# Expert phase of a routed MLP: two tiles of one expert taken together, their up product with channels on partitions

## The reference

```python
def _moe2_ref(x, expert_emb, tau, w1, w2):
    # N, D, E, F = 3072, 384, 8, 1024
    xn = x / (norm(x) + 1e-6);  en = expert_emb / (norm(expert_emb) + 1e-6)
    logits = xn @ en.T / tau
    expert_idx = np.argmax(logits, axis=1)
    gate_w = softmax(logits)[arange(N), expert_idx]
    for e in range(E):
        mask = expert_idx == e
        h = np.maximum(x[mask] @ w1[e], 0.0)
        out[mask] = gate_w[mask, None] * (h @ w2[e])
```

## Time and profile before

| what | value |
|---|---|
| median of 3 runs | 976.58 us (976.44 to 978.68) |
| the profiled execution | 976.46 us, its span 974.7 us |
| granted clock of TensorE, mean | 0.961 |
| TensorE busy | 862.5 us (88%) |
| VectorE, ScalarE, GpSimd busy | 661.7, 464.9, 503.7 us |
| expert phase | from 657.1 us (first transposes of x) to the end |

### The profile page before, as it was taken

The page is one execution under the profiler, slowest core; times in us unless marked ns, Lnnn a source line. Parts: engine busy times, 40 slices in busy tenths (PEclk is TensorE's granted clock), DMA queues, the critical chain, the costliest instruction groups (busy, mean ns, idle before and its releaser), DMA issues.

```text
span 974.7 us, 18389 instructions
## 1 busy us (share of the span) xinstructions
PE 862.5 (88%) x6398; PEld 766.3 (79%) x6399; DVE 661.7 (68%) x1058; ACT 464.9 (48%) x859; POOL 503.7 (52%) x884
## 2 busy tenths in 40 slices
PE   1658897889989999999999999839999999999995
PEld 1435786778879888888898889828888888888785
DVE  5968897889898998999876664276232343556621
ACT  5775754645645666655454432134232333456531
POOL 1294989699998988889890000012222223233221
PEclk9968999999999999999999999968999999999998
DMA  9201152343424243231411110345311141416310
GB/s 314 91 20 30 46 142 70 87 112 90 117 70 104 86 127 83 76 86 57 109 44 46 39 38 20 140 155 202 128 42 32 48 163 41 170 43 224 104 42 31
DMA packets 41799, 89.36 MB, mean 92 GB/s; under 512 B 6248, under 2 KB 23664, under 8 KB 40416
## 3 DMA queue, kind: packets, MB, share of 16 engines
q1 hardware_dynamic: 37632, 76.04, 25.3%
q0 software_dynamic: 4096, 12.40, 4.0%
HBM read 69.55 MB, written 17.69 MB: 90 GB/s over the span
## 4 chain that ended last, share of the span: by engine, by line
PE 60%; DVE 21%; ACT 7%; issue 7%; DMA 3%; SPq 2%; DVEq 0%; POOL 0%; ACTq 0%; POOLq 0%
PE mm L1597 7%; PE mm L1601 6%; PE mm L1598 6%; PE yu L1597 5%; PE tr L1597 4%; PE tr L1601 4%; PE tr L1598 4%; PE yu L1598 4%; PE yu L1601 4%; PE mm L1837 3%; PE sc L1654 3%; PE yu L1695 2%; DVE l_im L1099 2%; DVE l_re L1098 2%; DVE h_sb L1118 2%
## 5 line engine op out<-in xcount | busy, mean ns | idle before, releaser
L1597 PE MATMUL mm<-up_hi,x_hi 128*128 128x384 f32 x432 | 157.7, 365 | 30.5 <-DVE h_sb L1118 14.8
L1598 PE MATMUL mm<-up_lo,x_hi 128*128 128x384 f32 x432 | 148.2, 343 | 0.0
L1917 POOL TENSOR_TENSOR c_re<-ring 112x128 f32<-112x128 f32 x165 | 97.5, 591 | 79.8 <-DVE ring L1071 48.0
L1995 POOL DMA_INDIRECT out_rows<-g_o,rows_out x30 | 34.7, 1155 | 179.7 <-DVE g_o L1514 179.7
L1918 POOL TENSOR_TENSOR c_im<-ring 112x128 f32<-112x128 f32 x165 | 120.4, 730 | 0.0
L1597 PEld LDWEIGHTS mm<-up_hi,x_hi 128*128 128x128 f32 x432 | 82.3, 190 | 46.3 <-DVE h_sb L1118 18.1
L958 ACT ACTIVATE g_h<-tr 128x512 f32<-128x512 f32 x60 | 35.9, 598 | 171.3 <-PE tr L1601 169.8
L1601 PE MATMUL mm<-up_hi,x_lo 128*128 128x384 f32 x432 | 100.5, 341 | 0.0
L1921 POOL TENSOR_TENSOR ring<-c_re,c_im 112x64 f32<-112x64 f32 x165 | 98.4, 596 | 0.0
L1973 POOL DMA_INDIRECT g_in<-x_scratch,rows_in x33 | 37.3, 1130 | 102.1 <-DVE rows_in L1463 77.6
L1920 POOL TENSOR_TENSOR ring<-c_re,c_im 112x64 f32<-112x64 f32 x165 | 80.3, 486 | 12.9
(11 more groups left out here) (244 smaller groups left out, 2111.0 us busy)
## 6 DMA issues: line engine op xcount, KB each, us to landing
raw<-in_moe_w SPq DMA_DIRECT2D x16, 1536.0 KB, 8.8
a_dn<-in_a_laid SPq DMA_DIRECT2D x18, 384.0 KB, 6.8
an_scratch<-a_dn SPq DMA_DIRECT2D x18, 384.0 KB, 2.3
ring<-an_scratch SPq DMA_DIRECT2D x18, 384.0 KB, 5.5
q_in<-in_q_laid SPq DMA_DIRECT2D x24, 224.0 KB, 3.1
k_in<-in_k_laid SPq DMA_DIRECT2D x24, 224.0 KB, 3.2
v_in<-in_v_laid SPq DMA_DIRECT2D x24, 192.0 KB, 3.3
x_scratch<-x_sb SPq DMA_DIRECT2D x24, 192.0 KB, 2.5
```

What stands on the lines that cost most here:

```text
L1597: nc.tensor.matmul(out, hi[:, x, :], w_hi(x), start=(x == 0), stop=False)
L1598: nc.tensor.matmul(out, hi[:, x, :], w_lo(x), start=False, stop=False)
L1917: nc.gpsimd.tensor_tensor(c_re[:, 0:count, :, :], cur, bc(prev[:, :, 0, :], 2, 2), ALU.mult).then_inc(chain_prod, 1)
```

## The change

An expert's tiles are taken in pairs; a tile left over, an expert of one tile and tile 0 are taken by `single`, which is the tile of before with another read-ahead. A pair of tiles t and t+1:

- TensorE computes h transposed: the stationary operand is a block of 128 channels of w1 and the moving one the x of both tiles, 256 columns. 8 blocks x 9 matmuls write 4 banks (`tr` and `mm`). h then has its channels on partitions, as the down product wants it, so h isn't transposed. The down product is made per tile, into `ub` and `yb`.
- ScalarE writes `gh_hi` with the Relu straight out of the bank, VectorE makes `gh_lo` with the maximum and the subtraction in one instruction. 4 of each per pair.
- Both x must be ready when a pair begins. `gx_hi` and `gx_lo` hold two tiles, `g_x` two banks, and x is read two tiles ahead. In a single, the second tile's x is copied to the first place, on ScalarE and on VectorE.
- GpSimd's step for tile t is now: gather tile t+3, wait for its landing and post `g_here`, then `store_tile(t)`.
- The gates product moves ahead of tile 0, since the one-hot tiles' memory is used again by the tiles of x and h.

The diff, cut to its core:

```diff
@@ ScalarE
-            def expert_tile(t, split=None):
+            def single(t, split=None, very_first=False):
...
-                gx_high(t + 1)
+                if very_first:
+                    gx_high(1, 1, 0)
+                    gx_high(2, 0, 1)
+                else:
+                    nc.scalar.activation(gx_hi[:, :, 0, :], gx_hi[:, :, 1, :].bitcast(F32), ACT.Copy).then_inc(high_passed, 1)
+                    act.wait_ge(high_passed, t)
+                    gx_high(t + 2, 1, 1)
...
+            def pair(t, split=None):
+                act.sem_inc(gh_ready, 4)
+                act.sem_inc(high_passed, 2)
+                for b in range(4):
+                    act.wait_ge(gh_done, 2 * t + b + 1)
+                    if b == 0:
+                        act.wait_ge(go_done, t)
+                    nc.scalar.activation(gh_hi[:, 2 * b:2 * b + 2, :, :].rearrange("p k s t -> p (k s t)"),
+                                         (tr if b < 2 else mm)[:, b % 2, :], ACT.Relu).then_inc(ghh_ready, 1)
...
+                gx_high(t + 2, 0, 0)
+                gx_high(t + 3, 1, 1)
@@ VectorE
+            def scale(t, y):
+                dve.wait_ge(go_done, t + 1)
+                dve.wait_ge(go_free, t + 1)
+                nc.vector.tensor_scalar(g_o[:, ds(t % 2, 1), :].rearrange("p t d -> p (t d)"), (ub, yb)[y][:, 0:HD], table_gate[:, ds(t, 1)], None, ALU.mult) \
+                    .then_inc(go_ready, 1)
...
+            def pair(t, split=None):
+                dve.sem_inc(low_passed, 2)
+                gx_move(t + 2, 0, t + 2)
+                if split is not None:
+                    split_lo(split, 0)
+                for b in range(4):
+                    if b == 2:
+                        gx_move(t + 3, 1, t + 2)
+                    dve.wait_ge(ghh_ready, 2 * t + b + 1)
+                    part = slice(2 * b, 2 * b + 2)
+                    nc.vector.scalar_tensor_tensor(gh_lo[:, part, :, :].rearrange("p k s t -> p (k s t)"), (tr if b < 2 else mm)[:, b % 2, :], 0.0,
+                                                   gh_hi[:, part, :, :].rearrange("p k s t -> p (k s t)").bitcast(F32), ALU.max, ALU.subtract) \
+                        .then_inc(ght_ready, 1)
+                gx_low(t + 2, 0, 0)
+                gx_low(t + 3, 1, 1)
+                if split is not None:
+                    split_lo(split, 1)
+                    split_lo(split, 2)
+                scale(t, 0)
+                if split is not None:
+                    split_lo(split, KX)
+                scale(t + 1, 1)
+                if split is not None:
+                    split_lo(split, KX + 1)
@@ TensorE
+            def pair(t, e, x_slot, new):
...
+                pe.wait_ge(ght_ready, 2 * t)
+                pe.wait_ge(gxh_ready, t + 2)
+                pe.wait_ge(gxt_ready, t + 2)
+                x_hi, x_lo = (tile[:, :, :, :].rearrange("p k s t -> p k (s t)") for tile in (gx_hi, gx_lo))
+                for f in range(KG):
+                    out = (tr if f < 4 else mm)[:, f // 2 % 2, f % 2 * 2 * P:(f % 2 + 1) * 2 * P]
+                    rows = slice(f * P, (f + 1) * P)
+                    for x in range(KX):
+                        w_hi, w_lo = (tile[:, x_slot, x, rows] for tile in (e1_hi, e1_lo))
+                        nc.tensor.matmul(out, w_hi, x_hi[:, x, :], start=(x == 0), stop=False)
+                        nc.tensor.matmul(out, w_lo, x_hi[:, x, :], start=False, stop=False)
+                        last = nc.tensor.matmul(out, w_hi, x_lo[:, x, :], start=False, stop=(x == KX - 1))
+                    if f % 2 == 1:
+                        last.then_inc(gh_done, 1)
+                pe.sem_inc(ght_done, 4)
+                fetch_x(t + 2, 0, t + 2)
+                fetch_x(t + 3, 1, t + 2)
+                pe.wait_ge(go_ready, t)
...
+                for y in range(2):
+                    product((ub, yb)[y][:, 0:HD], gh_hi[:, :, y, :], gh_lo[:, :, y, :], lambda x: e2_hi[:, slot, x, :], lambda x: e2_lo[:, slot, x, :], KG,
...
@@ GpSimd
                 held(g_fetched[x], 16 * (pair + 1))
                 pool.sem_inc(g_here, 1)
-                held(gx_moved, t + 1)
-                fetch_tile(t + 2, x)
+
+            def fetch_next(t, x):
+                held(gx_moved, t - 1)
+                fetch_tile(t, x)
...
             def expert_tile(t, pair, x):
-                pass_on(t + 1, pair + x, 1 - x)
+                fetch_next(t + 3, 1 - x)
+                pass_on(t + 3, pair + x + 1, 1 - x)
                 store_tile(t, pair, x)
```

More of the change, by code:

```diff
@@ L1526, in expert @@
-                with dve.If(end - begin > 1):
-                    with dve.Fori(begin + 1, end) as t:
-                        expert_tile(t)
-            gx_move(0)
-            gx_low(0)
+                split = e + 1 if not isinstance(e, int) else None
+                count = end - begin
+                with dve.If(count > 1):
+                    pair(begin, split)
+                    with dve.If(count > 3):
+                        with dve.Fori(begin + 2, end - 1, 2) as t:
+                            pair(t)
+                    with dve.If(count % 2 > 0):
+                        last = dve.value_load(tiles_i[0:1, 2, ds(e, 1)], min_val=1, max_val=SLOTS - 4)
+                        single(last)
@@ L1532, in _ @@
+                with dve.If(count < 2):
+                    single(begin, split)
+            gx_move(0, 0, 0)
+            gx_low(0, 0, 0)
             for n in range(KX, PIECES):
                 split_lo(0, n)
-            expert(0)
+            end = dve.value_load(tiles_i[0:1, 1, 0:1], min_val=1, max_val=SLOTS - 3)
+            single(0, 1, very_first=True)
+            with dve.If(end > 2):
+                with dve.Fori(1, end - 1, 2) as t:
+                    pair(t)
+            with dve.If((end + 1) % 2 > 0):
+                last = dve.value_load(tiles_i[0:1, 2, 0:1], min_val=1, max_val=SLOTS - 4)
+                single(last)
@@ new lines, in expert @@
+            def expert(e, x_slot):
+                begin = pe.value_load(tiles_i[0:1, 0, ds(e, 1)], min_val=1, max_val=SLOTS - 4)
+                end = pe.value_load(tiles_i[0:1, 1, ds(e, 1)], min_val=1, max_val=SLOTS - 3)
+                count = end - begin
+                with pe.If(count > 1):
+                    pair(begin, e, x_slot, True)
+                    with pe.If(count > 3):
+                        with pe.Fori(begin + 2, end - 1, 2) as t:
+                            pair(t, e, x_slot, False)
+                    with pe.If(count % 2 > 0):
+                        last = pe.value_load(tiles_i[0:1, 2, ds(e, 1)], min_val=1, max_val=SLOTS - 4)
+                        single(last, e, False)
+                with pe.If(count < 2):
+                    single(begin, e, True)
@@ new lines, in _ @@
+            pe.wait_ge(tiles_ready, 1)
+            fetch_x(0, 0, 0)
+            end = pe.value_load(tiles_i[0:1, 1, 0:1], min_val=1, max_val=SLOTS - 3)
+            single(0, 0, True, very_first=True)
+            with pe.If(end > 2):
+                with pe.Fori(1, end - 1, 2) as t:
+                    pair(t, 0, 0, False)
+            with pe.If((end + 1) % 2 > 0):
+                last = pe.value_load(tiles_i[0:1, 2, 0:1], min_val=1, max_val=SLOTS - 4)
+                single(last, 0, False)
@@ L1866, in _ @@
+            with pe.Fori(1, E // 2) as double:
+                for x in range(2):
+                    expert(2 * double + x - 1, 1 - x)
+            expert(E - 1, 1)
         @block.gpsimd
@@ L2007, in _ @@
             pass_on(1, 0, 1)
+            fetch_next(2, 0)
+            pass_on(2, 1, 0)
+            fetch_next(3, 1)
+            pass_on(3, 1, 1)
             pool.wait_ge(table_made, 2)
```

172 lines of the change are left out of this document (97 added, 75 removed).

## The result

| | median us | lowest to highest |
|---|---|---|
| changed kernel, 4 runs | 1003.06 | 1002.89 to 1004.85 |
| kernel before, 4 runs | 977.13 | 976.44 to 978.68 |

What follows compares the result with a forecast made beforehand. It expected the loop of scaling, gather and landing wait (19.5 us a pair) to bound pairs instead of TensorE. 976.5 + 3.6 for the summed terms + 7.4 for low clock = 987 us; range 962 to 1003.

Steps and rivals of the forecast that it cites:

- TensorE's work in a pair: Up, remaining x transposes and down on TensorE: 17.4 us a pair against 19.78, -28.6 us for 12 if TensorE stays the bound.
- dear columns: Rival: in up, 256-column matmuls cost more than half of 512; at 0.174 us each a pair takes 21.5, total 997; chance 0.05.
- TensorE staying the bound: Rival: gathers land within about 2 us or the loop holds less; all 12 pairs save 2.4 us, total 949; chance 0.12.
- The wait that replaces the transposes: GpSimd's landing wait makes 7.1 us turns; a pair takes 19.5 us, TensorE standing about 2 us between up and down.
- The sum: All terms over the kernel: +3.6 us without the clock, then +7.4 for low clock, giving 987 us.
- pair 1 and the start: Gates product ahead of tile 0 leaves -0.5 us; the pair at tile 1 meeting the first loads adds 0.
- pairs 3 to 11 and 20: Pairs following a pair without a load between: -0.25 us each before the clock, -1.8 for seven including tile 27's.
- pair 27: Last expert's pair following a pair, counted among seven ordinary ones: -0.25 us before the clock.
- pairs 13 and 18, with a load: Second pairs of experts 1 and 2: a load delays the needed gather, 4.2 us more each on the loop, +8 together.
- pairs 16 and 25, after a single: Pairs following a single, where the loop has time in hand: 2 x -2.4 us, -4.8 together.
- singles of experts 4 to 6: VectorE's extra copy and wait, 3 x 0.45 = +1.4 us, plus +1.3 for expert 6's load holding the first.
- The clock: Stalls bring TensorE's half clock, 1.7 us lost each: one in three of seven ordinary, 4.0, and both load stalls, 3.4; +7.4.

Runs made afterwards that it cites:

- experiment 1: late_wait: changed kernel, GpSimd awaits each gather's landing one step after issuing it, each gather issued one tile further ahead; 951.03 us, ratio 0.9733.
- experiment 2: Changed kernel, GpSimd posts go_free and copies rows_out before the landing wait, the store staying behind it; 979.67 us, ratio 1.0030.
- experiment 7: Changed kernel with every tile taken as a single, GpSimd's program kept; 980.74 us, ratio 1.0053.
- experiment 9: Changed kernel, TensorE transposes a pair's second x between the down products, VectorE moves that x after all four low parts; 980.01 us, ratio 1.0033.
- experiment 10: filler: changed kernel with 18 unused 128-column matmuls per pair between TensorE's two x transposes; 1015.98 us, ratio 1.0411.
- experiment 3: no_loads: changed kernel without raw-weight loads of experts 2 to 7, which compute with weights of experts 0 and 1; 991.70 us, ratio 1.0157.
- experiment 4: small_split: no_loads, with VectorE making low parts of weights of experts 2 to 7 for only 8 columns; 983.21 us, ratio 1.0064.

## Why the prediction was right in kind and short in size

By its own steps:

- **TensorE's work in a pair**: forecast 17.4 us; the trace has 8.48 for up (0.118 a matmul of 256 columns, forecast 0.117), 0.65 and 8.41, together 17.54. Right: the rivals of dear columns and of TensorE staying the bound fall.
- **The wait that replaces the transposes**: forecast 19.5 us a pair, turns of 7.1 and 12.4. Where no half clock fell in, pairs 5 and 9 took 19.7 and 19.6 and pair 11 20.1 (its gather, issued beside a split, landed after 3.6 us), with turns of 7.2 to 7.3 and 12.4 to 12.5. Right, and shown by experiments 1, 2, 7 and 9.
- **The sum**. For each tile, how much later its down product starts than in the kernel before; a row is what that delay grew by over its places, a pair taken at its second down product. All in us; the last two columns are the share of half clock in each:

| place | forecast | measured | clock, forecast | clock, measured |
|---|---|---|---|---|
| pair 1 and the start | -0.5 | +1.96 | 0 | 1.56 |
| pairs 3 to 11 and 20 | +1.9 | +3.86 | 3.4 | 3.26 |
| pair 27 | +0.3 | +4.26 | 0.6 | 2.55 |
| pairs 13 and 18, with a load | +11.4 | +14.27 | 3.4 | 3.83 |
| pairs 16 and 25, after a single | -4.8 | -3.84 | 0 | 0 |
| singles of experts 4 to 6 | +2.7 | +5.93 | 0 | 1.76 |
| other singles | 0 | +1.21 | 0 | 0 |
| sum | +11.0 | +27.65 | 7.4 | 13.0 |

So two terms of the sum were too small. The clock came to 13.0 us against 7.4, a third of what was missing. The waits without the clock came to 14.7 against 3.6, spread over all places. Away from the two loads the forecast priced each landing at 3.1 us, and it added nothing to a turn for the splits; the trace has landings up to 4.1 us there, and turns of 8.0 to 9.0 us beside splits.

- **The clock, counted at too few places.** "I take one ordinary stall in three ... and both long ones: +7.4". Its price was right: 1.7 us a stretch forecast, 1.75 by experiment 10. One in three was nearly right too (pairs 5 and 11 of the six from 3 to 11 and 20), but half clock also fell on pair 1, pair 27 and expert 4's single. The products behind the seven holes are longer than 8.41 (or 4.32) by 1.56, 1.69, 1.57, 1.86, 1.97, 1.76 and 2.55 us. The long holes had 6.8 us of half clock each, but TensorE stood idle in a part of it, so the two at the loads cost 3.8 us, near the 3.4 forecast. I had one stall of 1.42 and one of 1.74 us to go by, and made of them a chance per ordinary pair instead of going through every place with a stall.
- **"The pair at tile 1 ... meets the loads of experts 2 and 3: 0"** was wrong: the hole is 2.85 us. Its step waits for a gather that lands in 6.3 us beside the first loads, as I had read for pair 13 and not applied here; the half clock followed.
- **Experts 4 to 6: "3 x 0.45 ... +1.3"** was too little, since I priced the single alone and not what the pair before it leaves. The scaling of pair 20's second tile waits for go_free, and the last but one split and the copy of x stand behind it. VectorE's timeline of the changed kernel:

```profile
904.28 0.62 DVE L1538 TENSOR_SCALAR g_o<-yu,table_gate 128x384 f32 x1 [6.45 <-POOLq L2129]
904.81 1.75 DVE L1403 TENSOR_TENSOR e_lo<-raw,e_hi  x1
907.88 0.36 DVE L1517 COPY g_x<-g_in 128x384 f32 x1 [1.31 <-issue]
```

TensorE's timeline, expert 4's single:

```profile
908.29 0.90 PE L1904 MATMUL sc<-ident,g_x 128*128 128x128 f32 x3 [3.90 <-DVE g_x L1517]
```

- **Pair 27 as an ordinary one**: its gathers land in 4.1 and 3.8 us, the hole is 3.55 us and a stretch of 6.8 us at half clock begins within it. The kernel before has landings of 3.7 to 3.9 us in its last tiles too, where nothing waited for them.
- **The loads**: pairs 13 and 18 were forecast at +8 without the clock and 11.4 with it, and measured 10.4 and 14.3. The landings were shorter than the 7.3 us that I took (6.1 and 6.8), but GpSimd itself is slower beside VectorE's splits (last section), a term that the forecast did not have: 1.38 us in the hole of pair 13 by experiments 3 and 4.
- **The range** ended at 998 + 5. Its 998 counted half clock in seven ordinary pairs and two long ones, 18 us. The clock cost 13, and the waits made up for it with 11 more than forecast. That the end of the range came within 0.1 us of the result is luck.

The Trainium skill (TensorE: Matmul & The Clock Gate, HAM oscillation) tells of a loop with waits of 3 to 5 us that falls back to the low clock each turn; in the changed kernel all four holes of over 3 us had it, and three of the seven between 1.5 and 2.9 us.

What stays open: which holes of 2 us bring the half clock (2.03 did, 2.05 and 2.58 did not), and whether late_wait's gain splits evenly into holes and clock; no run has the holes without the clock over the whole phase.

## What to carry to other kernels

When work is taken in pairs, each step that another engine makes per tile comes twice behind a pair's work, close together: compare the two steps with what lies over the second alone, not with the pair's total. A wait for a transfer that the same step has just issued puts its landing into every turn of a queue; put one step between issue and wait, as late_wait does, and 3 us a turn are gone (26 us slower became 25 us faster). And before a wait is moved, list what stands behind it in each queue that it passes, VectorE's as well as GpSimd's, at the boundaries of experts above all, since that is where holes, loads and the clock meet.

## What the runs showed of the hardware

- GpSimd's indirect DMA instruction takes 1.0 us, and as a store 1.68 us when it meets a split of weights on VectorE (two operands and a result in SBUF); this held for every such store of the changed kernel. Gathers that met a split took 1.0 to 1.8 us. Two stores in GpSimd's timeline of the changed kernel, the second beside the split at 904.81:

```profile
884.09 0.99 POOL L2133 DMA_INDIRECT out_rows<-g_o,rows_out  x1 [1.39 <-DVE g_o L1538]
...
905.75 1.68 POOL L2133 DMA_INDIRECT out_rows<-g_o,rows_out  x1 [1.52 <-DVE g_o L1538]
```

The turns beside splits are 8.0 to 9.0 us in the place of 7.2. With the splits cut to 8 columns (small_split) the stores of those tiles take 1.0 us and the turns 7.4 to 8.2. The Trainium skill (SBUF — State Buffer, Who interferes with whom) has VectorE instructions with two SBUF inputs contend with GpSimd instructions that read SBUF; the trace agrees, with 0.68 us.

- In filler TensorE's program grew by 18 instructions in each of its pairs' copies; the trace has 60 instruction packets against 50, and at three changes of experts a branch in TensorE's own program took 3.5 to 6.6 us (4.8 ahead of the row at 880.17) while some of them arrived. In the changed kernel no branch of its expert phase takes over 0.4 us. That the program's size is the cause was not tested by itself.
- A gather of 192 KB lands in 3.0 to 4.1 us without loads (no_loads, most in 3.0 to 3.2). Issued within 5 us of a load of 3 MB it lands in 5.8 to 8.1, over all kernels with loads.
